# Attention sums spread by two transfers, an earlier load of q and k, and one unsplit fp32 product for the last key tile

## The reference, cut to what matters

```python
# attention, B=2, H=8, S=768, D=64, 16 centroids per head
mask   = argmax(q_n @ c_n) == argmax(k_n @ c_n)      # same cluster
scores = where(mask, q @ k.T / sqrt(D), -1e9)
attn   = exp(scores - max(scores));  attn /= sum(attn) + 1e-9
x      = attn @ v                                    # -> (1536, 512)
# first MLP, 512 -> 2048 -> 512
h = x @ w_in;  x = (relu(h) + alpha * min(h, 0)) @ w_out
# second MLP, same sizes, a ratio of polynomials instead of relu
h = x @ w_in2; x = (P(h) / (Q(h) + 1e-6)) @ w_out2
```

## Time and profile before

| what | value |
|---|---|
| median of 3 runs | 864.3 us (860.86 to 866.19) |
| the profiled execution | 865.32 us |
| its span in the trace | 863.5 us |
| mean granted clock of TensorE | 0.981 |
| busy: TensorE, VectorE, ScalarE, GpSimd | 809.2, 604.2, 514.2, 300.9 us |

### The profile page before, as it was taken

The page is one execution under the profiler, slowest core; times in us unless marked ns, Lnnn a source line. Parts: engine busy times, 40 slices in busy tenths (PEclk is TensorE's granted clock), DMA queues, the critical chain, the costliest instruction groups (busy, mean ns, idle before and its releaser), DMA issues.

```text
span 863.5 us, 13502 instructions
## 1 busy us (share of the span) xinstructions
PE 809.2 (94%) x4339; PEld 753.8 (87%) x4339; DVE 604.2 (70%) x1019; ACT 514.2 (60%) x1043; POOL 300.9 (35%) x324
## 2 busy tenths in 40 slices
PE   5889898898999998999999999998999999999996
PEld 4779787787798998999999999997998998988895
DVE  6878788887878543344443344458888888888885
ACT  2667677776777710111111113367999999999995
POOL 3466868777677559800000005662000000000000
PEclk9989999999999998999999999998999999999999
DMA  6434463454533223400000003430000000001001
GB/s 175 125 100 130 109 157 103 102 147 103 141 93 77 69 68 98 123 0 0 0 0 0 0 1 95 125 111 11 2 1 37 0 0 36 0 0 37 0 1 38
DMA packets 30079, 52.17 MB, mean 60 GB/s; under 512 B 8944, under 2 KB 11088, under 8 KB 30032
## 3 DMA queue, kind: packets, MB, share of 16 engines
q1 hardware_dynamic: 30032, 51.59, 21.8%
HBM read 29.40 MB, written 3.19 MB: 38 GB/s over the span
## 4 chain that ended last, share of the span: by engine, by line
PE 61%; DMA 11%; DVE 10%; POOL 9%; ACT 5%; issue 3%; SPq 1%; POOLq 0%; ACTq 0%; DVEq 0%
PE work L191 26%; PE acc L872 14%; PE acc L880 13%; DMA scratch<-spread 6%; DVE row_max L776 3%; DVE probs_lo L281 2%; DMA op_b<-neg_max 2%; PE work L540 2%; POOL probs_lo L281 2%; DMA raw<-in_qk 2%; DMA stage<-in_moe_w_in 1%; PE work L514 1%; PE scores L568 1%; POOL head_hi L399 1%; POOL w_lo_b L1020 1%
## 5 line engine op out<-in xcount | busy, mean ns | idle before, releaser
L197 ACT ACTIVATE g_hi<-g_f 128x384 fp32r<-128x384 f32 x128 | 67.4, 527 | 223.4 <-PE acc L872 208.0
L209 DVE TENSOR_SCALAR corr<-work,alpha_c 128x384 f32<-128x384 f32 x64 | 39.5, 617 | 141.4 <-PE work L191 141.3
L649 ACT ACTIVATE probs_hi<-scores 128x384 fp32r<-128x384 f32 x192 | 94.9, 494 | 55.5 <-PE scores L568 52.4
L281 DVE TENSOR_TENSOR probs_lo<-probs,probs_hi 128x384 fp32r<-128x384 f32 x128 | 98.8, 775 | 38.0 <-ACT probs L652 37.0
L191 PE MATMUL work<-x_hi,w_hi_b 128*128 (+1 forms) x352 | 119.6, 340 | 3.6 <-POOL w_lo_b L1020 3.6
L191 PE MATMUL work<-x_lo,w_hi_b 128*128 (+1 forms) x352 | 119.5, 340 | 0.0
L191 PE MATMUL work<-x_hi,w_lo_b 128*128 (+1 forms) x352 | 119.5, 339 | 0.0
L652 ACT ACTIVATE probs<-scores 128x384 f32<-128x384 f32 x192 | 94.6, 493 | 15.6 <-POOL probs_lo L281 12.6
L776 DVE TENSOR_REDUCE row_max<-work 128x1 fp32r<-128x768 f32 x96 | 88.5, 946 | 4.7 <-PE work L540 4.5
L281 POOL TENSOR_TENSOR probs_lo<-probs,probs_hi 128x384 fp32r<-128x384 f32 x64 | 68.8, 1075 | 41.4 <-ACT probs L652 41.3
L201 DVE TENSOR_TENSOR g_lo<-g_f,g_hi 128x384 fp32r<-128x384 f32 x128 | 77.7, 607 | 0.6 <-ACT g_hi L197 0.6
(11 more groups left out here) (131 smaller groups left out, 2112.0 us busy)
## 6 DMA issues: line engine op xcount, KB each, us to landing
stage<-in_moe_w_in SPq DMA_DIRECT2D x27, 256.0 KB, 2.6
stage<-in_moe_w_out SPq DMA_DIRECT2D x27, 256.0 KB, 2.9
raw<-in_qk SPq DMA_DIRECT2D x16, 384.0 KB, 3.5
op_a<-head_hi SPq DMA_DIRECT2D x32, 192.0 KB, 3.1
v_raw<-in_v SPq DMA_DIRECT2D x16, 192.0 KB, 3.5
op_b<-head_hi SPq DMA_DIRECT2D x16, 192.0 KB, 3.1
op_b<-head_lo SPq DMA_DIRECT2D x16, 192.0 KB, 3.3
scratch<-spread SPq DMA_DIRECT2D x8, 384.0 KB
```

The lines of the kernel that those rows point to most:

```text
L281: eng.tensor_tensor(probs_lo[:, g % P_RING], probs[:, g % F_RING], probs_hi[:, g % P_RING].bitcast(F32), ALU.subtract).then_inc(pool_lo_ma ...
L649: act.activation(probs_hi[:, g % P_RING], s, ACT.Exp, scale=SCALE).then_inc(exp_hi_made, 1)
```

## The change

Four things change.

- `spread_recip` and the same step behind attention use two transfers of 64 rows, one for each head of the pair, with a semaphore each, where there was one transfer with a source of the shape [2, 64, S].
- The order of SyncE's queue: `load_qk(n + 3)` now comes first in head n, where it came after `put_max(n + 1)`; the copies come next and `move_sums(n - 1)` after them.
- The units of the last key tile, u = 5 and 11 (`FULL`), are no longer split. ScalarE makes one fp32 exponential into `probs_full`, and TensorE adds one fp32 matmul with `v_full`, which a new DMA `load_v_full` fills from the input. Its other 64 columns are set to ones by two new memsets on VectorE. No rest is made for these units.
- The rests of `POOL_LO = (2, 6, 9)` are GpSimd's; VectorE makes the other seven of ten.

```diff
+        FULL = (T - 1, 2 * T - 1)
+        POOL_LO = (2, 6, 9)
...
+                def load_v_full(m):
+                    e = m % 2
+                    at_least(sp, pv_made, (m - 1) * U)
+                    sp.dma_start(v_full[:, e, e * D:(e + 1) * D], v[m][:, (T - 1) * D:T * D]).then_inc(v_full_loaded[e], 16)
...
-                    sp.dma_start(rb, spread[p % 2].unsqueeze(1).to_broadcast([2, 64, S])).then_inc(recip_spread, 16)
+                    for e in range(2):
+                        sp.dma_start(rb[e * 64:(e + 1) * 64], spread[p % 2, e].partition_broadcast(64))\
+                          .then_inc(recip_spread[e], 16)
...
                 for n in range(N):
-                    if n >= 1:
-                        move_sums(n - 1)
+                    if n + 3 < N:
+                        load_qk(n + 3)
                     if n + 2 < N:
                         copy_a(n + 2)
                         copy_b(n + 2)
+                    if n >= 1:
+                        move_sums(n - 1)
+                    if n + 1 < N:
+                        load_v_full(n + 1)
                     if n % 2 == 0 and n >= 2:
                         put_recip(n // 2 - 1)
                     if n + 1 < N:
                         put_max(n + 1)
-                    if n + 3 < N:
-                        load_qk(n + 3)
...
-                    make_lo(pool, g + POOL_LO[3])
...
+                    if u in FULL:
+                        pe.wait_ge(exp_made, g + 1)
+                        pe.wait_ge(v_full_loaded[e], 16 * (n // 2 + 1))
+                        pe.matmul(to, v_full[:, e], probs_full[:, FULL.index(u)], start=False, stop=(kt == T - 1))\
+                          .then_inc(pv_made, 1)
+                        return
...
+                    if u in FULL:
+                        at_least(act, pv_made, g + 1 - U)
+                        act.activation(probs_full[:, FULL.index(u)], s, ACT.Exp, scale=SCALE).then_inc(exp_made, 1)
+                        return
...
+                    dve.memset(v_full[:, e, (1 - e) * D:(2 - e) * D], 1.0).then_inc(v_set, 1)
```

More of the change, by code:

```diff
@@ L92, in build @@
         v_loaded = sem("v_loaded")
+        v_full_loaded = [sem(f"v_full_loaded{e}") for e in range(2)]
         w_loaded = [sem(f"w_loaded{u}") for u in range(2)]
@@ L125, in build @@
         recip_row = sem("recip_row")
-        recip_spread = sem("recip_spread")
+        recip_spread = [sem(f"recip_spread{e}") for e in range(2)]
         x_made = sem("x_made")
@@ L161, in build, with split_units @@
         UNITS = N * U
-        POOL_LO = (2, 5, 8, 10)
+        FULL = (T - 1, 2 * T - 1)
+        POOL_LO = (2, 6, 9)
         H_RING = 4
+        SPLIT = U - len(FULL)
+        def split_units(g):
+            return g // U * SPLIT + g % U - sum(x < g % U for x in FULL)
         def at_least(eng, semaphore, value):
@@ L235, in build @@
             probs_lo = sba("probs_lo", [P, P_RING, HS], F32R)
+            probs_full = sba("probs_full", [P, len(FULL), HS])
+            v_full = sba("v_full", [P, 2, 2 * D])
             stage_a = sba("stage_a", [P, 2, DM])
@@ L276, in wait_lo, with unit_of @@
                     before = sum(x in POOL_LO for x in range(u))
-                    at_least(eng, dve_lo_made, n * (U - len(POOL_LO)) + (u - before + 1))
+                    at_least(eng, dve_lo_made, split_units(g) + 1 - n * len(POOL_LO) - before)
             def make_lo(eng, g):
+                k = split_units(g)
                 eng.wait_ge(exp_made, g + 1)
-                eng.tensor_tensor(probs_lo[:, g % P_RING], probs[:, g % F_RING], probs_hi[:, g % P_RING].bitcast(F32),
+                eng.tensor_tensor(probs_lo[:, k % P_RING], probs[:, k % F_RING], probs_hi[:, k % P_RING].bitcast(F32),
                                   ALU.subtract).then_inc(pool_lo_made if g % U in POOL_LO else dve_lo_made, 1)
+            def unit_of(k):
+                return k // SPLIT * U + [u for u in range(U) if u not in FULL][k % SPLIT]
             def bits(ap):
@@ L350, in _ @@
                 load_v(0)
+                load_v_full(0)
                 copy_a(0)
@@ L443, in scale_x @@
                     if a == 0:
-                        pool.wait_ge(recip_spread, 16 * p + 16)
+                        for e in range(2):
+                            pool.wait_ge(recip_spread[e], 16 * p + 16)
                     pool.tensor_tensor(xu[:, p % 2, cols], xu[:, p % 2, cols], rb[:, cols], ALU.mult).then_inc(x_made, 1)
@@ L573, in weigh @@
                     e, a, kt = n % 2, u // T, u % T
[L574 removed]
+                    to = pv[:, a, 0:HS]
+                    if u in FULL:
[4 more added lines that the diff above has]
+                        return
+                    k = split_units(g)
+                    pe.wait_ge(exp_hi_made, k + 1)
                     if u == 0:
@@ L799, in _ @@
                     late = 2 if n == 0 else 0
-                    if g >= 1 and (g - 1) % U not in POOL_LO:
+                    if g >= 1 and (g - 1) % U not in POOL_LO + FULL:
                         make_lo(dve, g - 1)
```

20 lines of the change are left out of this document (10 added, 10 removed).

## The result

The changed kernel takes 854.28 us (median of 4 runs, 853.52 to 857.67) where the kernel before takes 865.25 (4 runs beside it): a ratio of 0.989, with a 95% interval of 0.9845 to 0.9935. It is about 1% faster, by 11 us where I had forecast 24. The profiled execution took 857.67 us, with a span of 855.9 and a mean clock of 0.983.

What follows compares the result with a forecast made beforehand. No engine is full in attention, so waits between engines bound it; the terms sum to -24.5 us, taking the profiled 865.3 us to 840.8 and the median to about 840, range 825 to 854.

Steps and rivals of the forecast that it cites:

- step h: SyncE's queue: sums behind the eight copies make the inverses later in seven even heads; bounds 0 and +14 us, taken +5.
- The sign that I had named against myself: VectorE standing at `invert_sums` for the sums by more than 1 us a head would speak against the forecast.
- b: Lower clock in attention: 15.9 us busy, which at full clock would be half; bounds -8.0 and 0, taken -4 us.
- Rival 4: Slower: sums behind the copies close a circle in even heads, a loss if GpSimd's split begins late; 873 us, chance 0.04.
- c: GpSimd's late rests in attention, caused by the spread and by q and k: bounds -14.3 and -5, taken -11 us.
- a: TensorE's waits for the row maxima in attention, 8.2 us now, go without a spread in flight: -8 us.
- e: Behind attention: TensorE's 3.6 us wait for the weight load and half the lower clock behind it go: -6 us.
- Rival 3: The spread is no faster, by the skill's rule or because 64 reads of one row serialize: 864 us, chance 0.06.
- d: One rest a head fewer on VectorE, two exponentials fewer on ScalarE: bounds 0 and -11.6, taken -5 us.
- f: TensorE's fp32 product: two passes for each of two instructions, +0.17 us for each of 32 units, taken +4.
- g: Start-up: two memsets on VectorE and one DMA issue ahead of the first copies; between 0 and +1, taken +0.5 us.
- Rival 1: Waits just move to VectorE and the chain exponential, rest, product; half of a, b, c stays: 852 us, chance 0.15.

Runs made afterwards that it cites:

- e1: The changed kernel with only `move_sums` put back ahead of the copies: 838.46 us, ratio 0.9668 to the kernel before.
- e3: The kernel before with only `move_sums` moved behind the eight copies: 885.83 us, ratio 1.0216.
- e6: The changed kernel with `invert_sums` moved from u = 8 to u = 9, behind the cluster marks: 856.28 us, ratio 0.9929.
- e7: The changed kernel with `put_max` ahead of `put_recip` in SyncE's queue: 853.91 us, ratio 0.9893.
- e14: The changed kernel with `move_sums` ahead of the copies in the odd heads only: 854.04 us, ratio 0.989.
- e9: The changed kernel with `invert_sums` behind the cluster marks and `put_max` ahead of `put_recip`: 846.68 us, ratio 0.9774.
- e13: e9 with `move_sums` ahead of the copies in the odd heads only: 836.63 us, ratio 0.9697 to the kernel before.
- e2: The kernel before with only the spread made as two transfers of 64 rows: 844.24 us, ratio 0.9757.
- e4: e2 with the load of q and k one head earlier, first in the queue: 845.36 us, ratio 0.979 to the kernel before.
- e10: e1 with `load_qk(n + 3)` put back behind `put_max(n + 1)`: 838.5 us, ratio 0.9701 to the kernel before.
- e5: The kernel before with only the unsplit units 5 and 11 and POOL_LO = (2, 6, 9), old queue and spread: 869.21 us, ratio 1.0051.

## Why the prediction was wrong, step by step

The direction and the mechanism of the gain were right, and the time was just above the range of 825 to 854, because **step h (SyncE's order) failed**. I had taken it at +5 us with bounds of 0 and +14. It measured 16 us by the medians of the changed kernel and e1, 19 by their ratios, past even the dear end. (The 20 us of e3, in the kernel before, go largely by another path, ScalarE's.) The sign that I had named against myself came: VectorE stood at `invert_sums` for 6.7 us in five heads, 1.3 each. Three things in the step were wrong.

- *The paths.* I followed the sums on one path, `invert_sums`, `put_recip`, `put_max`, and priced how much later the inverses are written. Two others start there: the marks behind `invert_sums` on VectorE, for which TensorE then waits, with the lower clock behind the wait (b comes back in another place), and `take_pv` on ScalarE, which waits for the same `sums_moved` in the odd heads. I had charged nothing for either. The first costs the changed kernel its time together with the one that I had; the second holds up nothing in it yet, but takes the rest as soon as both are closed. e6, e7, e14 gain nothing, e9 half, e13 all.
- *The landing.* I had the inverses issued 2.6 to 3.6 us behind the sums. In head 6 it was 2.7 us (141.53 to 144.23), in head 8 it was 4.7 (174.13 to 178.81), and the loss is in heads like the second.
- *The cover.* I named "that GpSimd, no longer held by the spread, starts the split earlier (in head 8 it began 2 us into the head)". It began at 165.46 in a head that starts, by its first products on lines 585 and 595, near 163: over 2 us in, as before. Its odd head ends with the rest of u = 9 and the split of the attention output, whatever the spread does.

Rival 4 described one circle of the three and gave it 0.04, because it asked for a late start of the split before it priced a loss. What the lengths of heads show is milder than its 873 and worse than my +5. The issues of the maxima mark them; in the changed kernel:

```profile
159.86 0.75 SPq L348 DMA_DIRECT2D op_b<-neg_max  x1
...
196.00 0.76 SPq L348 DMA_DIRECT2D op_b<-neg_max  x1
```

and in e1:

```profile
155.24 0.76 SPq L348 DMA_DIRECT2D op_b<-neg_max  x1
...
186.80 0.76 SPq L348 DMA_DIRECT2D op_b<-neg_max  x1
```

Head 8 and the odd one behind it run from 159.86 over 179.31 to 196.00, 19.5 and 16.7 us; in e1 they run from 155.24 over 172.10 to 186.80, 16.9 and 14.7. In the kernel before the odd one took 15.2, from 180.81 to 196.05. The loss is in some heads, not in all: heads 4, 8 and 12, each with the odd one behind it, are together 15.9 us longer than in e1, of 16.7 us between the two profiled executions, while heads 6, 7, 10 and 11 together are only 2.1 longer. The long ones are those with the wait of 2.17 us and a stretch at 1.2 GHz behind it.

The other terms:

- Without h my sum was -29.5, a ratio of 0.966; e1 measured 0.9668, and attention ends there near 285, as I had said. The sum held better than its terms, and that is partly luck: what the load of q and k did not give, the unsplit units gave.
- My reading that the chain runs through one spread was wrong: it runs through four, and the other three took over 13 us each. So c and a rested on a slower transfer than I had counted with.
- *a, b, e and the spread's half of c* came to -24. e2 measured -21.6. e is seen by itself: no wait near 330 and full clock there, some 5 us of the span (7.6 less the 2.9 of attention). Rival 3 (the spread no faster, 864) is out.
- *c, the half of q and k* (-5) was worth nothing: e4 against e2 and e1 against e10. The intervals of the two pairs together leave room for some 4 us. This wait was off the path, which the total of a list of waits doesn't say.
- *d and f* together were -1, and the unsplit units measured -5 to -10 on top of the fast spread, alone +4.4 by the ratio. The size of f itself was right: the pair took 0.65 us where I had 0.69 by two passes each for two instructions, +0.13 for each of 32 units, 4.2 us. So by difference d, with the rests of GpSimd that fall away, was worth more than the 5 that I gave it, in a kernel where nothing else was late.
- *g*: no cost is seen in the first head, whose maxima are issued at 23.29 us against 23.46 before.
- Rival 1 (half of the gains stays, 852) has a time near the measured one for the wrong reason: with the sums in time the gains are all there.

What stays open: why the sums' transfer took 3.4 us in heads 4, 8 and 12 and 2.2 in heads 6 and 10, with the same bytes and the same place in the queue. In the changed kernel these are the long heads, and the transfer takes as long there in e7 and e14 too. The chain of the changed kernel has both, heads 6 and 8:

```profile
141.53 2.16 DMA sums<-rows
...
174.13 3.45 DMA sums<-rows
```

Nor is it settled by how much each path would lengthen a head if it were the only one.

## What to carry to other kernels

Before a transfer is moved behind others in an in-order queue, list every instruction on every engine that waits for its semaphore, also those that wait only for its buffer to come free, and follow each to what is queued behind it. Where one such path hides behind another, closing one or two of them shows nothing or half, and this is no evidence against them; an experiment has to undo the common cause (e1) or close all (e13). And a wait of an engine is a gain only if what it does next is awaited: 26 us of waiting for q and k went and the time didn't move.

## What the runs showed of the hardware

- A broadcast whose source had the shape [2, 64, S] took 10.24 to 14.06 us in the chain of the kernel before, and two transfers of 64 rows with the same bytes landed within 3.1 to 4.1 us of their issue. Alone in flight the one had a DMA share of 0.13, two engines of 16, at 51 GB/s; the pair 0.78, at 283 GB/s. The Trainium skill's "DMA: Bandwidth & Descriptors", Rules for kernel authors, says both that two transfers to disjoint halves should be one and that an outermost dimension of two keeps a transfer on two engines at most. The trace agrees with the second, and where the one transfer has such a shape the measurement decides against the first.
- A slow transfer slowed those behind it: the maxima and the weight load took 6.22 and 11.04 us, and the sums of the even heads 8.2 in the median, where e2 has 2.1. With the spread fast TensorE's waits for the maxima fell from 8.2 to 3.7 us (e2), and with it slow and the heads shorter they rose to 15.7 (e5), and fell to 3.7 with the fast one in the same kernel (e10).
- A true fp32 product of 384 columns takes 0.65 us from start to end in the chain at full clock, as two instructions, where one of fp32r takes 0.17: 3.8 times as long, and 1.26 times the three that it replaces.
- A wait of 2.17 us of TensorE at the turn of head 8 was followed by 3.4 us at 1.2 GHz, one of 1.04 us at the turn of head 6 by full clock. With the sums in time there was less of it in the whole kernel: the mean clock was 0.983 in the changed kernel, 0.991 in e1 and 0.994 in e13.
